# FFT filter and two MLP layers on one core: the input loaded over all 128 partitions from a padded layout, in first groups of two rows

## What is computed

```python
X = np.fft.rfft(x, axis=1)
y = np.fft.irfft(X * (filt_r + 1j * filt_i)[None], n=3008, axis=1)   # (2, 3008, 256)
t = y.reshape(6016, 256)
h = t @ moe_w_in;   t = np.maximum(0.01 * h, h) @ moe_w_out          # 256 -> 2048 -> 256
h = t @ moe2_w_in;  r = np.maximum(h, 0.0);  return (r * r) @ moe2_w_out
```

## Time and profile before

| | |
|---|---|
| median of 3 runs | 1114.54 us (1111.32 to 1115.14) |
| profiled execution | 1113.61 us |
| its span | 1111.8 us |
| PE busy | 1096.1 us |
| VectorE, ScalarE, GpSimd busy | 776.9, 569.4, 301.5 us |
| mean granted clock of PE | 0.998 |

### The profile page before, as it was taken

One profiled execution on the slowest core, in us unless ns is written; L12 is line 12 of the kernel. 1 busy time (PEld: TensorE's weight loads), 2 busy tenths in 40 slices (PEclk: granted clock), 3 DMA queues, 4 the chain that ended last, 5 costly groups with the idle time before them and its releaser, 6 DMA issues.

```text
span 1111.8 us, 14506 instructions
## 1 busy us (share of the span) xinstructions
PE 1096.1 (99%) x5312; PEld 930.3 (84%) x5312; DVE 776.9 (70%) x1193; ACT 569.4 (51%) x991; POOL 301.5 (27%) x292
## 2 busy tenths in 40 slices
PE   6999999999999999999999999999999999999998
PEld 6899978888888888888888888888888888888887
DVE  1788788776777677667676676667666776676665
ACT  2455656455555455555554454454554554554443
POOL 0579743233234324233221121120120220210000
PEclk9999999999999999999999999999999999999999
DMA  9665110011211211211244300000000000000000
GB/s 233 181 204 155 54 48 1 1 43 36 65 50 47 48 50 50 51 43 50 67 129 139 116 1 1 38 1 1 38 1 1 36 1 1 39 1 1 39 1 35
DMA packets 63702, 58.21 MB, mean 52 GB/s; under 512 B 40720, under 2 KB 51088, under 8 KB 63632
## 3 DMA queue, kind: packets, MB, share of 16 engines
q1 hardware_dynamic: 63488, 57.10, 17.5%
q10 hardware_dynamic: 144, 0.20, 0.1%
HBM read 39.58 MB, written 17.69 MB: 52 GB/s over the span
## 4 chain that ended last, share of the span: by engine, by line
PE 95%; DMA 1%; SPq 1%; DVE 1%; issue 0%; POOL 0%; ACT 0%; DVEq 0%
PE PS L889 15%; PE PS L888 15%; PE PS L890 15%; PE PS L896 13%; PE PS L898 13%; PE PS L897 13%; PE PS L808 2%; PE PS L820 2%; PE PS L841 2%; DMA X<-in_x 1%; SPq L205 1%; PE PS L797 1%; PE PS L830 1%; PE PS L779 1%; POOL YF L381 0%
## 5 line engine op out<-in xcount | busy, mean ns | idle before, releaser
L583 ACT ACTIVATE GH<-GF 128x512 fp32r<-128x512 f32 (+1 forms) x384 | 238.8, 622 | 225.3 <-DVE GF L728 116.3
L734 DVE TENSOR_TENSOR GL<-GF,GH 128x512 fp32r<-128x512 f32 (+1 forms) x384 | 259.8, 682 | 108.0 <-ACT GH L583 101.3
L889 PE MATMUL PS<-GL,WOH 128*128 128x512 f32 (+1 forms) x768 | 296.3, 386 | 0.0
L888 PE MATMUL PS<-GH,WOH 128*128 128x512 f32 (+1 forms) x768 | 296.3, 386 | 0.0
L890 PE MATMUL PS<-GH,WOL 128*128 128x512 f32 (+1 forms) x768 | 296.1, 386 | 0.0
L896 PE MATMUL PS<-XH,WIH 128*128 128x512 f32 (+1 forms) x672 | 260.1, 387 | 1.2 <-DVE GF L719 0.8
L898 PE MATMUL PS<-XH,WIL 128*128 128x512 f32 (+1 forms) x672 | 259.2, 386 | 0.0
L702 DVE TENSOR_TENSOR GF<-PS,GF 128x512 f32<-128x512 f32 (+1 forms) x96 | 65.3, 680 | 170.4 <-ACT GF L554 170.4
L889 PEld LDWEIGHTS PS<-GL,WOH 128*128 128x128 f32 x768 | 144.1, 188 | 27.7
L890 PEld LDWEIGHTS PS<-GH,WOL 128*128 128x128 f32 x768 | 144.1, 188 | 27.7
L888 PEld LDWEIGHTS PS<-GH,WOH 128*128 128x128 f32 x768 | 144.1, 188 | 27.6
(11 more groups left out here) (65 smaller groups left out, 1064.5 us busy)
## 6 DMA issues: line engine op xcount, KB each, us to landing
FL<-in_filt SPq DMA_DIRECT2D x32, 224.0 KB, 3.5
TB<-in_tab SPq DMA_DIRECT2D x32, 182.0 KB, 2.8
X<-in_x SPq DMA_DIRECT2D x22, 256.0 KB, 8.6
out_y<-YT SPq DMA_DIRECT2D x4, 1024.0 KB, 4.4
wi<-PWH SPq DMA_DIRECT2D x16, 224.0 KB, 2.5
wi<-PWL SPq DMA_DIRECT2D x16, 224.0 KB, 3.1
WIH<-wi SPq DMA_DIRECT2D x8, 448.0 KB, 3.5
WIL<-wi SPq DMA_DIRECT2D x8, 448.0 KB, 4.5
```

The costliest lines, as they stand in the source:

```text
L583: nc.scalar.activation(GH[:, g, 0:width(s)], GF[:, g, 0:width(s)], ACT.Copy).then_inc(g_hi[kind], 1)
L734: nc.vector.tensor_tensor(GL[:, g, 0:w], GF[:, g, 0:w], GH[:, g, 0:w].bitcast(f32), ALU.subtract).then_inc(g_lo[kind], 1)
L888: nc.tensor.matmul(acc, wh, xh, start=first, stop=False)
L889: nc.tensor.matmul(acc, wh, xl, start=False, stop=False)
```

## The change

The host packs `x` into rows: each `n1` gets 48 residues in place of 47, the last one zero, and the 48 are cut into two halves of 24, so that partition p = 2 * n1 + h holds residues 24h to 24h + 23 of `n1`. The array has the shape of the tile, `[128, B, 24, D]`. Each transfer covers all 128 partitions. Each sequence is loaded in 8 groups of 2, 2, 2, 2, 4, 4, 4 and 4 rows, each with a semaphore of its own, 16 transfers in place of 24. `over_n1` waits inside its loop over the four rows, at each row that starts a group, for half 0 only (half 1 of a chunk always follows its half 0). GpSimd's memset of the padding row and its semaphore go. The rows of the DFT matrix are permuted on the host to the new order of the partitions; the transpose and the output are as before.

```diff
+XG = (2, 2, 2, 2, 4, 4, 4, 4)
...
-        x_in = [[sem(f"x_in{b}{g}") for g in range(6)] for b in range(B)]
-        x_pad = sem("x_pad")
+        x_in = [[sem(f"x_in{b}{g}") for g in range(len(XG))] for b in range(B)]
...
-        MG = [4] * 6
...
+        X_START = [sum(XG[:g]) for g in range(len(XG))]
...
-            xv = x.rearrange("b (n r) d -> n b r d", r=N2)
-
             def load_x(b):
                 m = 0
-                for g, k in enumerate(MG):
-                    for h in range(2):
-                        n = min(k, N2 - MH * h - m)
-                        sp.dma_start(X[64 * h:64 * h + 64, b, m:m + n, :],
-                                     xv[:, b, MH * h + m:MH * h + m + n, :]).then_inc(x_in[b][g], 16)
-                    m += k
+                for g, n in enumerate(XG):
+                    sp.dma_start(X[:, b, m:m + n, :], x[:, b, m:m + n, :]).then_inc(x_in[b][g], 16)
+                    m += n
...
-            nc.gpsimd.memset(X[64:128, :, MH - 1, :], 0.0).then_inc(x_pad, 1)
-
-            pool.wait_ge(x_pad, 1)
             pool.wait_ge(p_ps, 1)
...
             def over_n1(c, half):
                 b, m0 = c // 6, 4 * (c % 6)
-                pe.wait_ge(x_in[b][c % 6], 32)
-                if m0 + 4 == MH:
-                    pe.wait_ge(x_pad, 1)
                 if c >= 2:
                     pe.wait_ge(n1_sb[half], c - 1)
                 for k in range(4):
+                    if half == 0 and m0 + k in X_START:
+                        pe.wait_ge(x_in[b][X_START.index(m0 + k)], 16)
                     mm = nc.tensor.matmul(PS[:, 4 + 2 * half + c % 2, 128 * k:128 * k + 128],
                                           X[:, b, m0 + k, half * 128:half * 128 + 128], DM[:, 0, :], start=True, stop=True)
...
-    dft = np.stack([d, d.T, np.eye(128)], axis=1)
+    by_n1 = d.reshape(2, N1, 128).transpose(1, 0, 2).reshape(128, 128)
+    dft = np.stack([by_n1, d.T, np.eye(128)], axis=1)
...
+    def pack_x(x):
+
+        rows = _np.zeros((B, N1, R, D), x.dtype)
+        rows[:, :, :N2] = x.reshape(B, N1, N2, D)
+        return rows.reshape(B, 2 * N1, MH, D).transpose(1, 0, 2, 3)
+
...
-        "x": inputs["x"],
+        "x": pack_x(inputs["x"]),
```

## The result

The changed kernel takes 1106.55 us (median of 5 runs, 1105.38 to 1106.98). The kernel before took 1111.82 in the runs beside it (1111.32 to 1115.14, 5 runs), and 1113.3 to 1113.4 in the three later series beside the experiments. The ratio is 0.9941, with a 95% interval of 0.9923 to 0.9959: 0.59% faster, 4.6 to 8.6 us. It is taken over all these runs and not from the two medians, which alone give 0.9953. Run once more beside later experiments, the same code gave 1106.55 against 1113.34, a ratio of 0.9934 (0.9920 to 0.9948). The profiled execution took 1106.98 us, its span is 1105.2: 6.6 us less in both than in the earlier trace rows and the table of before. The forecast was 1106 and a gain of 8.2 us.

A forecast was written before the change was run, and what follows sets the result against it. PE was busy 1096.1 of 1111.8 us, leaving mainly its waits for X and its lower clock to gain. Terms 6.8 + 1.4 = 8.2 us off the 1114.54 median gave 1106 us, range 1103 to 1111.

The forecast's parts named there:

- The time: Whole kernel: 1106 us, from a gain of 8.2 us off the median of three runs, 1114.54.
- What bounds it: Whole kernel: PE busy 1096.1 of 1111.8 us; only its idle time or slow running can be gained.
- The rate: Load of X: 382 GB/s with transfers over 128 partitions, instead of 248; X landed by 21.0 us.
- The rival of a backlog that keeps the rate down: Load of X: wide loads in a deep queue stay near 273 GB/s; 1110 to 1112 us, chance 0.10.
- The rival with no effect on the rate: Load of X: HBM sets 248 GB/s, so widening does nothing; 1112.4 or 1114.1 us, chance 0.05.
- The one with small packets: First four groups of each batch: 2 KB pieces slow the load to 231 GB/s; 1116 us, chance 0.04.
- The term of the stops and the clock: First DFT stage: without waits for X, first transpose at 26.2 instead of 33.05 us; 6.8 us gained.
- The part for the clock: Last group of the first DFT stage: its 16 matmuls took 3.52 us instead of 1.8; 1.7 us.
- The term of the start: Start of the first stage: two-row groups let PE start at 4.2 instead of 6.07 us; 1.4 us gained.
- the bound for the slow stretch: PE's first us: if the clock's rise stays near 9.2 us, 0.9 us are gained instead of 1.9.
- No new wait and no cost of the semaphores, the memset and the permuted rows: First stage: small groups add no wait; semaphores, dropped memset and permuted DFT rows each count zero.
- The later stages shift as a whole: Behind the first transpose: loads wait for PE, so the pattern shifts unchanged; chance 0.03 of an effect either way.

The follow-up runs named there:

- wide-only run: The changed kernel with six groups of four rows (12 transfers of 512 KB) in place of the small first groups: 1107.44 us, ratio 0.9949 to the kernel before.
- halves in the new layout: The changed kernel with each X transfer cut into one for partitions 0 to 63 and one for 64 to 127: 1114.80 us, ratio 1.0010.
- filled run of before: The kernel before with extra unused matmuls in TensorE's stops behind chunks 8, 9 and 10 of half 0: 1113.58 us, ratio 1.0001.

## Why the prediction was right, and where it was off

**The time: right, in part by luck.** 1106.55 us lies beside the forecast of 1106, but the gain was smaller than 8.2 us: 6.6 between the two profiled executions and 6.8 between the medians beside the repeated run. The forecast took it off 1114.54, the median of three runs, and later series put the kernel before at 1113.3 to 1113.4. A gain taken 1.4 us too large and a start taken 1.2 us too high cancel.

**What bounds it: right.** Only the waits for X and the clock behind them could be gained, and the gain stands complete at the first transpose (6.70 us there, 6.6 at the end).

**The rate: right.** 385 GB/s in 5 to 15 us against the 382 taken; X was there at 20.8 us against 21.0. That the landing fits so well is one execution: it came at 23.5 in the second profile, 0.3 us ahead of its use where the prediction saw 2. The wide-only run brings 5.9 us alone, and halves in the new layout bring none. The rival of a backlog that keeps the rate down is refuted for 128 partitions (411 GB/s with a full queue). The loads of `TB` and `FL` over 112 partitions stay slower behind it: 280 GB/s over 18 to 27 us in the changed kernel, which is mostly theirs; whether for the backlog or for their shape is not shown. The rival with no effect on the rate fell too. The one with small packets fell as well, though small groups cost some of the rate: 385 GB/s against 414 with the wide transfers alone.

**The term of the stops and the clock, 6.8 us: right.** From the eviction of chunk 5, half 1, to the first transpose it is 7.90 us now and was 14.64, a difference of 6.74. The part for the clock was put at 1.7; filling the stops shows 1.5. The 1.7 compared 3.52 us with two units of 1.8, but the 3.52 hold the 0.17 us that a group ends behind its last issue.

**The term of the start, 1.4 us: mis-sized, it measured about zero.** Two steps are behind it. PE's start was put at 4.2, with `DM` at 3.4 as before. `DM` came at 4.6: beside X transfers over all partitions it took 3.9 us instead of 2.6, and it was now the last to arrive. That costs 0.5 us. The larger miss is the bound for the slow stretch: "if the rise stays where it is, near 9.2 us" was the worst case I took, and the rise came later than that, near 10.6. PE worked 5.9 us at the lower clock, at 0.213 us for each instruction instead of 0.112, so about 2.8 us of it are lost; before it was 2.9 us and about 1.4. 1.39 us of earlier start less 1.4 is nothing, as chunk 5 shows. In the second profile of the changed kernel, with the rise near 9.1, the first transpose is 0.73 us earlier, so some of the term can be there in single executions. The medians agree with this: they are 6.8 us apart beside the repeated run, and 5.3 in the first comparison, where the five runs of before have a lower median (1111.82) than in any later series.

**No new wait and no cost of the semaphores, the memset and the permuted rows: right.** PE has no stop in the first stage.

**The later stages shift as a whole: right for both profiles of the changed kernel, but not in general.** The 0.03 for it was little: in the run with `DM` in two parts 1.0 us of the lead went between 50 and 110 us, and in the filled run of before 1.05. Stops before filter loads that landed late make up nearly all of both, 0.95 and 0.90 us.

## What to carry to other kernels

A queue of transfers that each cover partitions 0 to 63 or 64 to 127 moved 237 to 250 GB/s, and one of transfers that reach both halves (all 128 partitions, or every second one) 371 to 414; look at the partitions of a load before its size. An earlier first matmul is worth something only if neither the last landing nor the lower clock at the start takes it back, so ask of each microsecond at the start which of the two holds it. Before moving a load to another queue for a few tenths of a microsecond, look at which loads it will then run beside or ahead of: `WIF` on ScalarE's queue made the filter loads land up to 5.4 us after their issue and cost 3.4 to 4.1 us. And where a table of waits names an engine, compare its end with the landings: here it named ScalarE, and the loads were the later ones.

## What the runs showed that I had not expected

`DM`, 192 KB on another queue, issued at the same moment as the first X transfer, took 2.6 us to land beside transfers of 64 partitions, 3.9 beside 256 KB over 128 and 4.6 beside 512 KB over 128. The rate of the neighbour alone does not do it: beside the transfers over every second partition it took 2.5, with 316 GB/s moved from 2.3 to 4.6 us, where the wide-only run moved 321. So look at when the small load that gates the start lands. And TensorE's clock rose between some 3 and 6 us after its first matmul in different executions, so a single profile does not tell what an earlier start is worth.
